# Feed-forward layers in five tiles of tokens instead of six, with buffers laid out anew

## The reference

```python
# attention: batch 4, heads 8, sequence 576, head dimension 64
scores = q @ k.T / sqrt(64) + bias            # bias: a small network of the relative position
attn = softmax(scores);  x = attn @ v         # x: (2304 tokens, 512)
# first feed-forward layer, d_ff = 2048
h = x @ w_in;  x = (h * cos(h)) @ w_out
# second feed-forward layer, d_ff = 1536
xn = x / sqrt(mean(x * x) + 1e-6) * rms_g
g = xn @ w_gate;  out = (g * sigmoid(g) * (xn @ w_val)) @ w_out
```

## Time and profile before

| | |
|---|---|
| time, median of 3 runs (lowest, highest) | 1194.29 us (1193.71, 1194.73) |
| time of the profiled execution | 1191.96 us |
| its span, first to last instruction | 1190.1 us |
| granted TensorE clock, mean | 0.998 |
| PE busy | 1163.0 us (98%) |
| weight loads busy | 1079.9 us (91%) |
| DVE, ACT, POOL busy | 662.5, 493.2, 477.6 us |

### The profile page before, as it was taken

The page is one execution under the profiler, slowest core; times in us unless marked ns, Lnnn a source line. Parts: engine busy times, 40 slices in busy tenths (PEclk is TensorE's granted clock), DMA queues, the critical chain, the costliest instruction groups (busy, mean ns, idle before and its releaser), DMA issues.

```text
span 1190.1 us, 21722 instructions
## 1 busy us (share of the span) xinstructions
PE 1163.0 (98%) x7464; PEld 1079.9 (91%) x7464; DVE 662.5 (56%) x1554; ACT 493.2 (41%) x1032; POOL 477.6 (40%) x506
## 2 busy tenths in 40 slices
PE   5889999999999999999999999999999999999998
PEld 2367777777899999999999999999999999999998
DVE  7978888888889857566665786642020020200201
ACT  7977778778733433333333333112121111111211
POOL 0067777777775423425242453841111111111111
PEclk9999999999999999999999999999999999999999
DMA  6844435253134000000000010430000000000000
GB/s 198 286 130 150 153 99 179 82 191 102 45 110 127 15 1 1 0 0 0 0 0 0 0 53 18 133 89 28 1 13 14 0 26 0 0 26 0 26 0 27
DMA packets 46681, 69.10 MB, mean 58 GB/s; under 512 B 3857, under 2 KB 27569, under 8 KB 46641
## 3 DMA queue, kind: packets, MB, share of 16 engines
q1 hardware_dynamic: 46640, 68.61, 18.5%
HBM read 53.26 MB, written 15.34 MB: 58 GB/s over the span
## 4 chain that ended last, share of the span: by engine, by line
PE 61%; issue 28%; POOL 6%; DVE 2%; DVEq 1%; DMA 1%; ACT 0%; POOLq 0%; SPq 0%; ACTq 0%
PE banks L531 7%; PE banks L857 7%; PE banks L859 7%; PE banks L858 7%; PE bank L857 6%; PE bank L859 6%; PE bank L858 6%; PE bank L573 6%; PE bank L557 5%; POOL product_low L1469 5%; PE bank L579 2%; DVE hidden L237 1%; DVEq L237 1%; PE bank L553 1%; PE bias_ps L271 1%
## 5 line engine op out<-in xcount | busy, mean ns | idle before, releaser
L857 PE MATMUL banks<-x_high,w_high_rest 128*128 128x384 f32 x672 | 225.4, 335 | 0.0
L859 PE MATMUL banks<-x_high,w_low_rest 128*128 128x384 f32 x672 | 224.6, 334 | 0.0
L858 PE MATMUL banks<-x_low,w_high_rest 128*128 128x384 f32 x672 | 224.6, 334 | 0.0
L1469 POOL TENSOR_TENSOR product_low<-X,product_high 128x384 fp32r<-128x384 f32 x72 | 72.9, 1013 | 345.6 <-ACT product_high L1412 345.6
L1450 DVE TENSOR_TENSOR X<-X,banks 128x384 f32<-128x384 f32 x72 | 39.7, 552 | 299.6 <-PE banks L859 299.6
L1252 POOL TENSOR_TENSOR product_low<-g,product_high 128x384 fp32r<-128x384 f32 x96 | 103.2, 1075 | 221.4 <-ACT product_high L1125 221.2
L857 PE MATMUL bank<-product_high,w_high_rest 128*128 128x384 f32 x480 | 160.6, 335 | 0.0
L859 PE MATMUL bank<-product_high,w_low_rest 128*128 128x384 f32 x480 | 160.4, 334 | 0.0
L858 PE MATMUL bank<-product_low,w_high_rest 128*128 128x384 f32 x480 | 160.4, 334 | 0.0
L678 DVE CUSTOM_DVE_ANT_0 probs<-banks,bias 128x576 f32<-128x576 f32 (+1 forms) x160 | 119.6, 748 | 16.3 <-PE banks L531 7.4
L626 ACT ACTIVATE probs<-probs,by_row 128x576 f32<-128x576 f32 (+1 forms) x160 | 123.4, 771 | 8.8 <-DVE by_row L678 7.4
(11 more groups left out here) (118 smaller groups left out, 2516.0 us busy)
## 6 DMA issues: line engine op xcount, KB each, us to landing
raw_qk<-in_qk SPq DMA_DIRECT2D x32, 576.0 KB, 3.8
bias_scratch<-bias_stage SPq DMA_DIRECT2D x36, 288.0 KB, 3.2
bias<-bias_scratch SPq DMA_DIRECT2D x32, 288.0 KB, 3.3
w_raw<-in_w_out SPq DMA_DIRECT2D x28, 256.0 KB, 2.6
values<-in_v SPq DMA_DIRECT2D x16, 320.0 KB, 4.1
w_raw<-in_w_in SPq DMA_DIRECT2D x16, 256.0 KB, 2.8
out_t<-X SPq DMA_DIRECT2D x5, 768.0 KB, 3.6
w_raw<-in_w_gate SPq DMA_DIRECT2D x12, 256.0 KB, 3.0
```

Source lines behind the costliest of these rows:

```text
L857: nc.tensor.matmul(out, high, x_high, start=start, stop=False)
L858: nc.tensor.matmul(out, high, x_low, start=False, stop=False)
L859: return nc.tensor.matmul(out, low, x_high, start=False, stop=stop)
L1469: pool.tensor_tensor(sl[f % 2][:, :], s, sh[f % 2][:, :].bitcast(F32), ALU.subtract).then_inc(s_split, 1)
```

## The change

`NT` becomes 480, so that there are five tiles: four of 480 tokens and a last one of `NT_LAST` = 384. Every helper of the feed-forward layers gets the width of its tile as an argument; `widths_of(tile)` gives those of the tile behind, of this one and of the next. Since the last tile has another width, it leaves the loops, and on ACT and DVE the last but one is written out too (it prepares features of the last one's width). `NSUB` becomes 4, so that a block of the normalisation is 120 tokens (96 in the last tile).

To make room, `raw_qk` becomes one tensor on the right side that `turns`, `angle` and `g` use as well after attention; `ident` moves to the right side; the small tensors of the normalisation move into `small`; each pair of product buffers becomes one tensor; and the scratch that GpSimd reserves for DMAs is set to 1024 bytes. The output of the last but one tile is kept in its own block of `X`, which first has to be stored.

```diff
-NT = 384
-TILES_T = TOK // NT
+NT = 480
+TILES_T = -(-TOK // NT)
+NT_LAST = TOK - (TILES_T - 1) * NT
...
-SUB = P
-NSUB = NT // SUB
+NSUB = 4
+SUB = NT // NSUB
...
+def widths_of(tile):
+
+    return tuple(NT if t < TILES_T - 1 else NT_LAST for t in (tile - 1, tile, tile + 1))
...
-        self.raw_qk = [sb(ctx, f"raw_qk{h}", [P, 2, S], F32) for h in range(2)]
+        self.raw_both = sb(first_layer, "raw_qk", [P, 4 * S], F32, "right")
+        self.raw_qk = [self.raw_both[:, h * 2 * S:(h + 1) * 2 * S].rearrange("p (i s) -> p i s", i=2) for h in range(2)]
...
-    def means(self, pe, t):
-
-
+    def means(self, pe, t, n):
+
+        sub = n // NSUB
         pe.wait_ge(self.consts_ready, 2)
         pe.wait_ge(self.summed, (t + 1) * self.SQUARE_STEPS)
         for i in range(NSUB):
-            last = self.nc.tensor.matmul(self.rms_ps[0:SUB, i:i + 1], self.squares[0][:, i * SUB:(i + 1) * SUB],
+            last = self.nc.tensor.matmul(self.rms_ps[0:sub, i:i + 1], self.squares[0][:, i * sub:(i + 1) * sub],
                                          self.by_dm[:, :], start=True, stop=True)
...
-    def add_first_buffers(self, sb, ctx, quarter):
-
-
-        self.turns = sb(ctx, "turns", [P, NT], I32, "right")
-        self.angle = sb(ctx, "angle", [P, NT], F32, "right")
-        self.g = sb(ctx, "g", [P, NT], F32, "right")
...
+    def add_first_buffers(self, room, quarter):
+
+
+        turns, self.angle, self.g = (room[:, i * NT:(i + 1) * NT] for i in range(3))
+        self.turns = turns.bitcast(I32)
...
             for f in range(C1):
                 if not first and f < LAG1:
-                    down(t - 1, C1 - LAG1 + f, False)
+                    down(t - 1, C1 - LAG1 + f, False, back)
                 if first and f >= LAG1:
-                    down(t, f - LAG1, True)
+                    down(t, f - LAG1, True, n)
                 if not (first and f < FIRST_H):
-                    up(t, f, first)
+                    up(t, f, first, n)
...
-        with pe.Fori(1, T) as t:
-            tile(t, False)
+        with pe.Fori(1, T - 1) as t:
+            tile(t, False, widths_of(1))
+        tile(T - 1, False, widths_of(T - 1))
...
+    homes = [min(t + 1, T - 2) for t in range(T - 1)] + [T - 1]
...
-    nc = bacc.Bacc("TRN2", target_bir_lowering=False, num_devices=1)
+    nc = bacc.Bacc("TRN2", target_bir_lowering=False, num_devices=1, dynamic_dma_scratch_size=1024)
```

More of the change, by code:

```diff
@@ L652, in pair @@
                     act.wait_ge(mixed_copied, (feature * B + 1) * 2)
-                    features.high(act, 0, feature)
+                    features.high(act, 0, feature, NT)
         pair(0, 0, True)
@@ L705, in early_features @@
                 dve.wait_ge(mixed_copied, (k * B + 1) * 2)
-                features.high(dve, 0, k)
+                features.high(dve, 0, k, NT)
             elif s % NQ == 4:
-                features.low(dve, 0, 0, k)
+                features.low(dve, 0, 0, k, NT)
         def pair(n, parity, step, hp=None, made=None):
@@ L1075, in up, with down @@
                 pe.wait_ge(g_ready, t * C1 + (f + 1 - h_back[f]))
-            chunks.up(pe, h_ps[h_at[f]], 2 * f, t, f == 0).then_inc(h_ready, 1)
-        def down(t, f, first):
+            chunks.up(pe, h_ps[h_at[f]], 2 * f, t, f == 0, n).then_inc(h_ready, 1)
+        def down(t, f, first, n):
             if first:
@@ L1133, in free_of, with tile @@
             return (down_done, t * DOWNS) if f == 0 else (x1_ready, t * KC)
-        def tile(t, first, last):
+        def tile(t, first, last, widths):
+            back, n, ahead = widths
             for f in range(C1):
                 if not (first and f == 0):
-                    chunks.count_turns(act, h_ps[h_at[f]], t, f)
+                    chunks.count_turns(act, h_ps[h_at[f]], t, f, n)
                 if f == C1 - 1:
@@ L1189, in product, with tile @@
                 dve.wait_ge(g_split, t * C1 + f)
-            dve.tensor_tensor(g[:, :], angle[:, :], h_ps[h_at[f]][:, 0:NT], ALU.mult).then_inc(g_ready, 1)
-        def tile(t, first, last):
+            dve.tensor_tensor(g[:, 0:n], angle[:, 0:n], h_ps[h_at[f]][:, 0:n], ALU.mult).then_inc(g_ready, 1)
+        def tile(t, first, last, widths):
+            back, n, ahead = widths
             for f in range(C1):
@@ L1343, in _, with up @@
     def _(pe):
-        def up(t, f, which, first):
+        def up(t, f, which, first, n):
             if first:
@@ L1350, in up, with down @@
                 pe.wait_ge(s_ready, t * C2 + (f - 1))
-            chunks.up(pe, val_ps[f % 2] if which else gate_ps, U1 + 3 * f + which, T + t, f == 0 and which == 0
-                      ).then_inc(val_ready if which else gate_ready, 1)
-        def down(t, f, first):
+            chunks.up(pe, val_ps[f % 2] if which else gate_ps, U1 + 3 * f + which, T + t, f == 0 and which == 0,
+                      n).then_inc(val_ready if which else gate_ready, 1)
+        def down(t, f, first, n):
             if first:
@@ L1402, in tile @@
                     for k in ACT_PARTS:
-                        features.high(act, t + 1, k)
+                        features.high(act, t + 1, k, ahead)
                 act.wait_ge(s_ready, c1)
@@ L1443, in tile @@
                     for k in DVE_PARTS:
-                        features.high(dve, t + 1, k)
+                        features.high(dve, t + 1, k, ahead)
                     for k in range(KC):
-                        features.low(dve, T + t + 1, t + 1, k)
+                        features.low(dve, T + t + 1, t + 1, k, ahead)
                 dve.wait_ge(silu_ready, c1)
```

339 lines of the change are left out of this document (180 added, 159 removed).

## The result

The changed kernel takes 1198.22 us (median of 4 runs, 1195.97 to 1199.38) against 1194.00 us for the kernel before beside it (4 runs, 1192.31 to 1194.73). The ratio is 1.0037 with a 95% interval of 1.0025 to 1.0049: slower by 4.4 us by the ratio (4.2 by the medians), where 10.6 us less was forecast. It lies above the forecast's high end of 1189.5 us. The profiled execution of after took 1195.97 us, which is 1.77 more than its span.

A forecast was written before the change was run, and what follows sets the result against it. From 333 us on TensorE hardly waits, so time is the number of matmuls by their step. Terms of -10.9 + 0.1 + 0.25 + 0 - 0.1 = -10.65 us gave a median of 1183.7 us, range 1182.0 to 1189.5.

The forecast's parts named there:

- Matmuls of the two layers: Feed-forward matmuls: 816 fewer, each with a fixed 13.3 ns beside its columns, so 10.9 us less.
- rival A: Feed-forward matmuls: the step follows the columns, so little or no gain, median 1188.9 to 1194.5 us; chance 0.12.
- Placement: New tensor addresses: the slower matmuls with tail weights may stay or go, -0.9 to 0 us, taken as -0.1.
- Rival B: All 4080 matmuls: new placement costs each what the tail costs now, 3 to 4 ns; 1200.0 us at 4; chance 0.07.
- The third `up`: Sign at the feed-forward start: starts 1.2 us later, from two `first_h` of 12 steps x 40 ns, and 0.25.
- the end of attention: Last two attention pairs: longer DVE rounding and subtracting for tile 0 adds 0.25 us, range 0 to +0.74.
- the rounds of the normalisation: TensorE's rounds of means and spread: 6.1 us now, five rounds with four blocks after, taken as +0.1 us.
- POOL's subtraction: Chain of each chunk: about 1248 ns at 480 columns, 1.16 times that at 384; the chain's term was 0.
- rival C: Each chunk: TensorE waits for the chain, 0.3 us in a quarter of 140 chunks, 10.5 us, median 1194.2; chance 0.05.

The follow-up runs named there:

- the kernel with padded blocks: The changed kernel with every block of x_high, x_low and the product buffers given room for 512 columns (480 used): 1193.69 us, ratio 0.9999.
- the kernel of 512 columns: The changed kernel with four tiles of 512 tokens and a last one of 256 instead of 480 and 384: 1189.10 us, ratio 0.9961.

## Why the prediction was wrong

**Step "Matmuls of the two layers": failed.** It took 213.3 ns at 480 columns, the line through 288 and 384 columns drawn on. The fixed 13.3 ns is real at 256, 320 to 400 and 512 columns with equal starts, and false at 480, where equal starts give 216.7 and only a start 48 bytes in reached 213.3. 3264 x 3.33 = 10.9 us, which by chance equals the 816 x 13.3 ns saved; so the kernel with padded blocks stands at 0.9999, and its time looks like rival A. A's number was right and its law wrong. The check that I used, the slope between two widths, can't see a surplus that begins at a third; and its left end was off as well: 288 columns alone take 131.7 ns, not 133.3, and I explained the 0.39 us that said so away.

**Step "Placement": failed by 4.1 us.** It took -0.1 where +4.0 came, and kept 0 as its worst end, though the tail's rows had shown the effect and the diff changes the stride of the very blocks. Rival B named the mechanism; I set it aside because head and rest "lie far apart and both have 334 to 336": far apart they are, but equal modulo 256 bytes. Its size was taken from mean durations (3 to 4 ns) and for all matmuls; by steps it is (217.6 - 216.7) x 3264 = 2.9 us at 480 and 2.35 x 816 = 1.9 us at 384. Of these 4.8 us the tail's own 288 x 2.7 = 0.8 us were in before too, which leaves 4.0. Together 10.9 + 4.1 = 15.0 us, against the 14.8 between the 10.6 less of the forecast and the 4.2 more that were measured.

**The other terms held.** The third `up` came 1.0 us later (1.2 predicted), of which 24 x 44 ns are the longer `first_h`; nothing is left for the end of attention, and the first feed-forward matmul starts at 321.79 us (before: 321.83). Beyond ordinary steps, the rounds of the normalisation cost 5.9 us where they had cost 5.0 (the prediction had 6.1, and +0.1); 0.6 of the 0.9 more lie in one round, whose means took 1.39 us against 0.76 in each of the three rounds before it. The pauses without a round came to 0.5 us less. Both are near what one profiled execution can tell. POOL's subtraction took 1265 ns (1248 estimated), and rival C is false here: 1.6 us of waits.

**What stays open.** Why some widths and starts cost 1 to 7 ns a matmul is not known. Shown is that at 480 and 384 columns in aligned blocks the surplus is gone with 2-byte operands, that at 384 columns a start 128 bytes off costs and one 256 bytes off does not, and that 416 to 496 columns have a surplus even with equal starts. Not explained is why half of the blocks off by 128 bytes cost about as much (2.3 ns a matmul) as all of them (2.3 alone, 2.7 in the kernel), and why the product blocks 1920 bytes apart cost 2.2 ns at 384 columns and nothing at 480; a contention between the reads of weights and of the moving operand would fit, and is only argued. For a loop with other weights the good start has to be measured.

## What to carry to other kernels

When TensorE hardly ever waits, the kernel's time is count times step, so read the step from starts, and at the very width and addresses that the change brings: a row of 48 matmuls alone costs one run and would have shown 216.7 against 213.3. A mean that is 1% off for one tensor is not noise to be carried as a small term; ask what that tensor has (here its address modulo 256) and how many operands get it by the change. Measure a few widths before choosing one: tiles of 512 and 384 gained 0.86%, where tiles of 480 and 384 lost 0.37%.

## What the runs showed of the hardware

- At 384 columns, moving blocks whose start differs from the weights' by 128 bytes modulo 256 cost 2.3 ns a matmul in matmuls alone (175.7 against 173.4) and 2.7 in the kernel (176.0 against 173.3); a difference of 256 bytes costs nothing. A 32-byte shift costs 3.3 ns there, and 6 ns at 512 columns (233.1 against 227).
- The part of a step beyond N / 2.4 is 13.3 ns with 4-byte operands and equal starts at 256, 320 to 400 and 512 columns, and 2.5 ns with 2-byte ones at 384 and 480.
- A stream of 448 columns keeps the step that it began with: 206.5 or 202.7 ns by the width ahead of it.
- The start-up differs between profiled executions by more than this change is worth at that place. Windows of 50 to 92 us, of after and then of the kernel with all blocks padded:

```profile
50.00:92.00 42.00, 34.60 (x291) 25.56 (x285) 35.17 (x111) 31.48 (x68) 20.48 (x22) 0.96 0.52 162
```

```profile
50.00:92.00 42.00, 34.64 (x279) 25.48 (x279) 34.67 (x107) 29.93 (x64) 18.11 (x20) 0.88 0.53 162
```

With a granted clock of 0.88 in place of 0.96, TensorE gets 12 matmuls less done, and the third `up` of the padded kernel starts at 336.84 us against 333.97. The edit is not needed for it: the kernel of 512 columns, profiled twice, had 0.88 and 0.96 there and its third `up` at 337.48 and 335.52 us, while the stretch behind it took 847.35 and 847.31 us. So single profiled spans of these kernels compare to about 3 us, and the stretch behind the third `up` to less than one.
